# A gated decay recurrence and two MLPs in one kernel: where the decay chain runs, how far it is spread, and how its results are sorted

## What is computed

```python
# attention, per head (B=4, H=8, S=768, D=48), S_re and S_im start at zero
mag = sqrt(a_re**2 + a_im**2);  scale = minimum(mag, 0.999) / (mag + 1e-6)
ar, ai = a_re * scale, a_im * scale
for t in range(S):
    new_re = ar[t] * S_re - ai[t] * S_im
    new_im = ar[t] * S_im + ai[t] * S_re
    S_re, S_im = new_re + outer(k[t], v[t]), new_im
    y[t] = q[t] @ S_re
x = y laid out as (3072 tokens, 384)
# first MLP, d_ff 2048:  h = x @ w_in;  x2 = (h * clip(h + 3, 0, 6) / 6) @ w_out
# second MLP, d_ff 1024: out = ((x2 @ w1) * (x2 @ w2)) @ w3 @ w_out2
```

## Time and profile before

| | us |
|---|---|
| median of 3 runs | 1075.39 (1074.17 to 1079.45) |
| the profiled execution | 1078.01 |
| its span in the profile | 1076.2 |
| until the first g_sb (passes 0 and 1, attention of unit 0) | 133.8 |
| unit 0 | 99.9 |
| units 1 to 5 | 408.7 (86.9, 81.0, 79.9, 81.1, 79.8) |
| unit 6 (attention, no decay chain) | 66.4 |
| unit 7 (neither) | 54.6 |
| second MLP and end | 312.8 |

### The profile page before, as it was taken

One profiled execution on the slowest core, in us unless ns is written; L12 is line 12 of the kernel. 1 busy time (PEld: TensorE's weight loads), 2 busy tenths in 40 slices (PEclk: granted clock), 3 DMA queues, 4 the chain that ended last, 5 costly groups with the idle time before them and its releaser, 6 DMA issues.

```text
span 1076.2 us, 14778 instructions
## 1 busy us (share of the span) xinstructions
...
## 2 busy tenths in 40 slices
...
GB/s 346 137 97 113 168 44 111 68 85 117 66 89 95 84 86 98 84 94 96 78 85 113 70 51 98 37 229 1 52 1 57 2 59 1 59 1 59 1 30 31
DMA packets 85720, 85.85 MB, mean 80 GB/s; under 512 B 8208, under 2 KB 77968, under 8 KB 85648
## 3 DMA queue, kind: packets, MB, share of 16 engines
...
## 4 chain that ended last, share of the span: by engine, by line
issue 35%; PE 31%; POOL 21%; DVE 5%; SPq 2%; ACT 1%; DMA 1%; POOLq 0%; DVEq 0%; ACTq 0%
POOL gL L1309 12%; PE hb L913 9%; PE acc L935 7%; PE bQ L913 5%; PE bR L913 5%; POOL QKs L1297 4%; POOL QKs L1302 3%; PE bP L935 2%; DVE W L1147 1%; POOL woutL L364 1%; PE acc L792 1%; POOL W L1291 1%; POOL W L1289 1%; PE hb L772 1%; DVE W L1139 1%
## 5 line engine op out<-in xcount | busy, mean ns | idle before, releaser
L1309 POOL TENSOR_TENSOR gL<-g_sb,gH 128x384 fp32r<-128x384 f32 x128 | 156.1, 1219 | 355.9 <-ACT gH L1005 355.9
L772 PE MATMUL hb<-xHL,winH 128*128 128x384 f32 x768 | 173.1, 364 | 21.0 <-DMA xHL<-yHL 17.5
L1198 DVE SCALAR_TENSOR_TENSOR g_sb<-t_sb,hb 128x384 f32<-128x384 f32 x128 | 70.4, 550 | 237.5 <-POOL gL L1309 126.4
L772 PEld LDWEIGHTS hb<-xHL,winH 128*128 128x128 f32 x768 | 144.7, 205 | 24.9 <-DMA xHL<-yHL 18.4
L792 PE MATMUL acc<-gH,woutH 128*128 128x384 f32 x384 | 134.5, 350 | 31.8 <-POOL gL L1309 30.9
L1324 POOL TENSOR_TENSOR pL<-p_sb,pH 128x512 fp32r<-128x512 f32 x48 | 67.0, 1396 | 231.9 <-ACT pH L1067 231.9
L792 PE MATMUL acc<-gH,woutL 128*128 128x384 f32 x384 | 134.0, 349 | 0.0
L792 PE MATMUL acc<-gL,woutH 128*128 128x384 f32 x384 | 133.4, 347 | 0.0
L1015 ACT ACTIVATE t_sb<-hb,cst 128x384 f32<-128x384 f32 x128 | 74.4, 581 | 130.3 <-PE hb L772 129.8
L1005 ACT CAST gH<-g_sb 128x384 fp32r<-128x384 f32 x128 | 65.3, 510 | 146.9 <-DVE g_sb L1198 146.8
L792 PEld LDWEIGHTS acc<-gH,woutH 128*128 128x128 f32 x384 | 75.2, 196 | 36.4 <-issue 36.3
...
## 6 DMA issues: line engine op xcount, KB each, us to landing
...
```

Source lines behind the costliest of these rows:

```text
L772: mm = pe.matmul(o, w[:, kk * DF1 + ft * P:kk * DF1 + (ft + 1) * P], xv(u)[:, 2 * kk + part, :], start=(i == 0), stop=(i == 8))
L1198: dve.scalar_tensor_tensor(out=g_sb[:, :], in0=t_sb[:, :], scalar=6.0, in1=hb[n % 2][:, 0:UNIT], op0=ALU.min, op1=ALU.mult).then_inc(s["hs ...
L1309: pool.tensor_tensor(gL[:, (n % 3) * UNIT:(n % 3 + 1) * UNIT], g_sb[:, :], gH[:, (n % 3) * UNIT:(n % 3 + 1) * UNIT].bitcast(F32), ALU.subt ...
```

## The change

Six things, all in the first MLP's part of the program:

1. The products of q and k with the decays and the sine go from POOL to DVE; the squares of passes 2 and later go from POOL to ACT. POOL keeps gL and the low parts of the weights.
2. The angle stays in radians: the offset add (L1139) goes into the scans, which now add two tiles, and a multiplication by 1/pi on ACT comes behind them.
3. The chain is spread: squares at step 0, sums and scans at 4, 6, 7, decays at 8 and 9, products at 10 and 11, wrap at 12, trigonometry at 13, cosine at 14, sine at 15. Unit 0 takes two or three steps in slots 0 to 3 and 15.
4. From unit 0 on YU stands two slots behind S (three for one chunk of unit 0); unit -1 keeps three slots in a row.
5. All 64 blocks of w3 @ w_out2 are multiplied at once; w_out is loaded at slot 0 of unit -1 (before slot 8), and five pieces of the weights are split in unit 0.
6. q and k lie by chunk in QKs and QKc, so that the first two chunks of a pass are sorted by 5 DMAs a half, of double size, the cosine half as soon as it is ready; the third keeps 10. In pass 0 ACT issues the sine half's.

```diff
+        ORDER_W = (0, 4, 1, 5, 2, 6, 3, 7)
+        SPLIT_H = {(-1, 0): (0,), (-1, 8): (4,), (-1, 9): (1,), (0, 1): (5,), (0, 3): (2,), (0, 5): (6,), (0, 7): (3,), (0, 9): (7,)}
...
             if u == 0:
-                return ([(1, sl + 10)] if sl < 4 else []) + ([(2, sl - 2)] if sl >= 3 else [])
+                return {0: [(1, 10), (1, 11)], 1: [(1, 12), (1, 13)], 2: [(1, 14), (1, 15)],
+                        3: [(2, 0), (2, 1)], 15: [(2, 13), (2, 14), (2, 15)]}.get(sl, [(2, sl - 2)])
...
-        W3_MM = {-2: {5: 40}, -1: {0: 3, 1: 3, 2: 3, 3: 3, 4: 2, 5: 2, 6: 2, 7: 2, 8: 4}}
-        W3_COPY = {(-2, 14): (0, 1), (-2, 15): (2, 3, 4), (-1, 3): (5,), (-1, 6): (6,), (-1, 8): (7,)}
+        W3_MM = {-2: {5: FT2 * FT2}}
+        W3_COPY = {(-2, 9): (0, 1), (-2, 10): (2,), (-2, 11): (3, 4), (-1, 0): (5,), (-1, 1): (6,), (-1, 2): (7,)}
...
+        STAGE = {-1: ((0, 3, 6), (1, 4, 7), (2, 5, 8)), 0: ((3, 7, 11), (4, 8, 12), (6, 10, 13))}
...
-            first, step = {-1: (0, 3), 0: (4, 4)}.get(u, (1, 4))
-            j, r = divmod(sl - first - STAGE[stage], step)
+            at_ = STAGE.get(u, ((1, 5, 9), (2, 6, 10), (4, 8, 12)))[("TK", "S", "YU").index(stage)]
...
+            eng.dma_start(f[r:r + D, :, 0:3 * QK], b[0:D, :, :]).then_inc(done, 16)
+            eng.dma_start(f[r:r + D, :, 3 * QK:6 * QK], b[D:D2, :, :]).then_inc(done, 16)
+            eng.dma_start(f[r:r + P - D2, :, 6 * QK:8 * QK], b[D2:P, :, 0:2 * QK]).then_inc(done, 16)
...
-                        if t == 13:
-                            scatter(CPU * p)
-                            scatter(CPU * p + 1)
+                        if t == 14:
+                            scatter_pair(sp, p, 0)
+                        if t == 15 and p > 0:
+                            scatter_pair(sp, p, 1)
...
                 if t == 12:
+                    act.wait_ge(s["turns_summed"], KT * (p + 1))
+                    act.mul(W2[:, :], W1[:, :], float(1 / np.pi)).then_inc(s["turns"], 1)
+                if t == 13:
                     act.wait_ge(s["turns_wrapped"], p + 1)
...
+                if t == 15 and p == 0:
+                    scatter_pair(act, 0, 1)
...
+                    dve.tensor_tensor(part(QKs, 0), part(QKs, 0), tokens(AI), ALU.mult).then_inc(s["q_decayed"], 1)
...
-                    dve.scalar_tensor_tensor(out=W2[:, :], in0=W2[:, :], scalar=float(1 / np.pi), in1=W3[:, :],
-                                             op0=ALU.mult, op1=ALU.add).then_inc(s["turns"], 1)
...
-                        dve.tensor_tensor_scan(W1[:, o], ONE_C.broadcast_to([P, UNIT]), W2[:, o],
-                                               total[:, j:j + 1] if p % 2 else 0.0, ALU.mult, ALU.add).then_inc(s["turns_summed"], 1)
+                        dve.tensor_tensor_scan(W1[:, o], W2[:, o], W3[:, o], total[:, j:j + 1] if p % 2 else 0.0,
+                                               ALU.add, ALU.add).then_inc(s["turns_summed"], 1)
...
+                if t == 15:
+                    dve.wait_ge(s["sin_turns"], p + 1)
+                    for i in range(2):
+                        dve.tensor_tensor(part(QKs, i), part(QKs, i), tokens(W2), ALU.mult).then_inc(s["sin_rotated"], 1)
```

More of the change, by code:

```diff
@@ L59 @@
 FD = 10
+QUARTER_TURN = float(np.float32(np.pi / 4))
 ROUND = 1.5 * 2.0 ** 23
@@ L111, in mixer_mlp_kernel @@
         QKc = at("QKc", KT * CPU * QK)
-        F = [at(f"F{i}", H * QK) for i in range(2)]
+        F2 = at("F2", 2 * H * QK)
+        F = [F2[:, i * H * QK:(i + 1) * H * QK] for i in range(2)]
         Kc = at("Kc", DM + YM - D)
@@ L614, in load_q @@
                 else:
[L615 to L616 removed]
+                    sp.wait_ge(s["f_pair_dma"], 16 * FD * p)
+                    sp.wait_ge(s["f_last_dma"], 16 * FD * p)
                 sp.dma_start(qk(QKs)[:, :, 0:P], qk_src(p, 0)).then_inc(s["q_dma"], 16)
@@ L706, in _ @@
                         store_w3(i)
-                    if u == -1 and sl == 8:
+                    if u == -1 and sl == 0:
                         for i in range(PIECES // 2, PIECES):
@@ L711, in _ @@
                         if g % CPU == 0:
-                            scatter(g + 2)
+                            scatter_last(g // CPU)
                         if g + 2 < NC:
@@ L955, in pre @@
             def pre(p, t):
-                if t == 1 and p <= 1:
+                if t == 0:
                     act.wait_ge(s["a_dma"], 32 * (p + 1))
-                    if p == 1:
-                        act.wait_ge(s["sin_rotated"], 2)
+                    if p > 0:
+                        act.wait_ge(s["sin_rotated"], 2 * p)
                     act.activation(W2[:, :], AI[:, :], ACT.Square).then_inc(s["squares"], 1)
+                    if p > 0:
+                        act.activation(W1[:, :], AR[:, :], ACT.Square).then_inc(s["squares"], 1)
                 if t == 2:
```

189 lines of the change are left out of this document (89 added, 100 removed).

## The result

| | us |
|---|---|
| before, median of 4 runs beside it | 1076.01 (1074.17 to 1079.45) |
| after, median of 4 runs | 1019.91 (1018.55 to 1022.37) |
| ratio | 0.9478, 95% interval 0.9447 to 0.9508 |
| span of after in the profile | 1020.6 |
| until the first g_sb | 105.4 (133.8 before, 105 forecast) |

The kernel is 5.2% faster, 56 us, where 85 were forecast. The time lies in the range by its edge alone, 0.1 under the upper bound where the runs spread over 4, so that it fell inside is luck; and the table says where the other 30 went: the start came out at its number, unit 0 is 15 over it (and longer than before), units 1 to 5 together are 15 over it.

What follows compares the result with a forecast made beforehand. PE was taken as the bound, held up by waits for gL, AT and Ks and a DVE-bound start; 1076.2 - 29 (start) - 10 (unit 0) - 47 (units 1 to 5) = 990; range 965 to 1020.

Steps and rivals of the forecast that it cites:

- The start, -29: Time until the first g_sb: 105 instead of 133.8, by a shorter DVE path, earlier scores and earlier w_out loads.
- ACT's five issues: Pass 0's sine-half sorting: issues take 3.3, landing 2.3, scores at 58.4; help from ACT as second issuing engine worth 3.
- late spot: In unit -1, SP stores w3's last row before the third chunk's sorting; chunk 0's outputs are stored by 79.
- Unit 0, -10: Unit 0 takes 90 against 99.9, including bigger lumps of pass 1 and 2 for splits beside DVE.
- Units 1 to 5, 72.1 each: Each of these units: 66.4 + 3.6 + 1.4 + 0.7; five take 361 against 408.7.
- The base, 66.4: What a unit costs TensorE, read from unit 6, where PE is busy 66.40 of 66.40 us.
- Ks and AT, 1.7 and 4.2, gone: PE's waits in unit 3 for copies Ks (1.7) and masks AT at the outputs (4.2) disappear.
- gL behind the sine products, 3.6, gone: PE's wait for gL behind POOL's sine products, about 2.2 plus 1.4 of clock, goes as DVE takes them.
- gL behind the trigonometry, 3.6, stays: PE's wait for gL behind ACT's trigonometry in slot 13, 2.24 plus 1.4 of clock, remains.
- End of the unit, 1.4 and 0.7: New wait of 1.4 at the unit's first gemm2, behind ACT's squares; possible clock loss of 1.4, counted half.
- Scores of the first chunk: The pair's last sorting DMAs land at 13.4, PE wants them at 14.5: covered by 1.1, otherwise at most 2 late.
- B: Rival: chain stays late through the unit's end, by scans, squares or scores' DMAs; units 77, total 1015; chance 0.16.

Runs made afterwards that it cites:

- eleventh experiment: On the changed kernel, SP also issues pass 0's sine half of the sorting, which ACT issued: 1023.34 us, ratio 0.9497.
- tenth experiment: On the changed kernel, the blocks of w3 @ w_out2, their copies and w_out's loads stand as before the change: 1022.16 us, ratio 0.9494.
- the third: On the changed kernel, ACT issues the sine half's five sorting DMAs in every pass, not in pass 0 alone: 1031.54 us, ratio 0.9571.
- first experiment: On the changed kernel, a pass's first two chunks are sorted one by one, 5 single-size DMAs a half, own semaphores: 994.39 us, ratio 0.9208.
- ninth experiment: All weight pieces split before unit 0, on the kernel with chunks sorted one by one and the sine in slot 14: 977.31 us, ratio 0.9076.
- last experiment: Changed kernel plus single-chunk sorting, later first scores, closer unit 0 stages, sine in slot 14, second square in slot 1, weight splits moved: 960.37 us, ratio 0.8906.
- eighth experiment: On the changed kernel, outputs stand one slot behind the scores again from unit 1 on: 1021.55 us, ratio 0.9454.
- seventh experiment: On the changed kernel, q and k's products with the decays and the sine are POOL's again from pass 2: 1042.92 us, ratio 0.9663.
- first two experiments: Two separate edits of the changed kernel: first two chunks sorted one by one (994.39 us); first chunk's scores one slot later from unit 1 (997.48 us).
- fourth experiment: On the changed kernel, the squares of passes 2 to 7 are POOL's again, behind gL of slot 0: 1022.93 us, ratio 0.9487.

## Why the prediction was right, and where it wasn't

**The start, -29: right, at 105.4.** Its steps held: arctangent done 37.7 (37.2 forecast), scans 40.4 (39.9), cosine products 50.3 (49.9), sine 52.9 (52.6), gemm1 from 101.5 (x landed at 101). One did not: the first scores came at 62.5, not 58.4, because ACT's five issues took 4.9 (3.3 forecast) and the last landed 4.7 behind them (2.3). The late spot that the prediction named did not hide that 4.1: SP's wait for w3's row moves with the scores, as the eleventh experiment shows, and the outputs of chunk 0 were stored by 82.5 instead of 79. The delay was gone when the outputs of chunk 2 ended (95.4 for 95), so the steps of the chain between were forecast some 3 too long; which of them, no run shows. That the start hit its number is two errors that cancel. DVE's products for the sine:

```profile
50.27 2.62 DVE L1202 TENSOR_TENSOR QKs<-QKs,W 128x1152 f32<-128x1152 f32 x2
```

With no POOL work beside them both pairs take 2.6, where the earlier trace rows had 5.85 for the second. The 10 that the prediction gave to w_out's loads, behind the first scores, are borne out in size (10.7 by the tenth experiment, the order of w3's rows included). What it did not set against them is that making all of w3 @ w_out2 at once costs 8.2 ahead of the scores; it had the wait (34) in its steps, but not its price. The rest of the start, 25.9 of 28.4, is the decay chain and the sorting, which no run takes apart.

**ACT's five issues.** I priced the help of the second engine at 3 and wrote that the trace doesn't agree with "small". It is 1.1 by the eleventh experiment, and in the third ACT's issuing in every pass brought nothing. The traces side with the Trainium skill here ("DMA: Bandwidth & Descriptors", Issuing engines are not separate DMA queues): it says that a second engine saves only the time to initiate, usually small beside the DMA. The DMA engines read 0.99 busy while the sine half was under way.

**Unit 0, -10: wrong, +5.** Two steps of it failed. *Sorting*: nothing was put down for it; by the first experiment it is 105.2 - 98.3 = 7. The first scores come behind a wait of 3.9, and gemm1 of two slots on stands behind them in PE's order. *Splits*: "I add 2 for splits beside DVE". By the ninth experiment five pieces in unit 0 are 10.6, their own time on ACT and POOL included, which that run doesn't take apart. The part on DVE shows in the cosine products, with POOL's split beside them:

```profile
124.16 5.84 DVE L1198 TENSOR_TENSOR QKc<-QKs,W 128x1152 f32<-128x1152 f32 x2
```

```profile
123.26 3.46 POOL L398 TENSOR_TENSOR woutL<-woutL_raw,woutH 128x1536 fp32r<-128x1536 f32 x1 [0.38 <-ACT woutH L394]
```

5.84 for 2.62, while the split itself takes 3.46. In the first experiment's kernel PE is past slot 6 of unit 0 at 42 us, where I had 41, and the rest takes 56 instead of 49: there the capping of the logarithm on DVE took 3.18 (0.75 alone) and the scans 6.65 (2.64 alone), both under splits. The prediction had the row that says so, 8.93 for 2.65 in the earlier trace rows, used it for pass 0, where the splits went away, and not for unit 0, where they came.

**Units 1 to 5, 72.1 each: 75.2, by one step.** With chunks sorted one by one they take 72.2. Step by step:

- *The base, 66.4*: right, partly by luck. "PE is busy 66.40 of 66.40 us" was read as what a unit costs TensorE. But unit 6 of before starts at half clock, behind a wait of 3.56 for gL:

```profile
642.00:646.00 4.00, 4.00 (x14) 4.00 (x13) 0.56 (x1) 0.51 (x1) 1.34 (x2) 0.50 0.50 113
```

  and it has 508 matmul records where unit 3 has 529. In the first experiment unit 6 takes 62.2 at full clock. The two errors cancel: in the last experiment, at full clock, unit 3 keeps PE busy for 66.2 (532 records).
- *Ks and AT, 1.7 and 4.2, gone*: right. But of my two reasons for AT one does nothing (eighth experiment).
- *gL behind the sine products, 3.6, gone*: right, one wait for gL is left. Put back on POOL the products cost 3.2 a unit, but by another path, through ACT's squares (seventh experiment).
- *Products at 1.32 to 1.7*: right, 3.43 and 3.44 a pair. Here the row was the better guide than the rule of full exclusion in the Trainium skill ("SBUF — State Buffer", Who interferes with whom), by which I had put a unit at 73 to 74: with sorting out of the way it took 72.2. Under the weight splits it is otherwise, as unit 0 shows.
- *gL behind the trigonometry, 3.6, stays*: right. A wait of 2.10 and then 3.4 us at the level of 1.2 GHz,

```profile
428.65 0.52 PE L816 MATMUL acc<-gH,woutH 128*128 128x384 f32 x1 [2.10 <-POOL gL L1328]
```

```profile
428.80:432.20 3.40, 3.40 (x12) 3.40 (x13) 3.40 (x3) 0.99 (x2) 1.51 (x1) 0.50 0.21 87
```

  and it was 3.2 a unit when it was removed. "Stays" was right of this change and no law: one line moved ends it.
- *End of the unit, 1.4 and 0.7*: the wait for gH is 0.9 to 2.1, as forecast. POOL is busy 19.3 a unit, not 16: gL is stretched by DVE's products, 1.5 for 0.99, without being late by it.
- *Scores of the first chunk*, "the last 5 start at 7.7; 5 x 0.65 and 2.4 to land give 13.4": this is the step that failed. From the first issue of the sine half to the scores it took 445.94 - 436.72 = 9.2, not 5.65: the 0.65 was 0.6 to 1.4, and the 2.4 was 4.7. I had taken issue and landing times from DMAs of half the size, one after the other, and held them for those of a DMA of double size with the cosine half in flight. It is 3.6 late against a cover of 1.1. The wait was bounded at 2 and is 1.2 to 2.7, and I had put no clock loss behind it: 3.4 us at half clock are 1.7 more. Since the wait for gH grows when the one for F goes, the two net to 3 a unit.

The rival that came nearest is B, chain late through the end of the unit, at 1015: it named "the scores' DMAs" among three causes, and the first two experiments single it out. The scans were as forecast (3.42 and 3.54). The squares cost nothing that shows while F is late (fourth experiment); with F there, a square moved to slot 1 goes with slots 0 and 1 falling from 7.3 to 6.4 (last experiment). The total lies 0.1 inside the range, with unit 0 and units 1 to 5 both 15 over; the start, right by errors that cancel, kept it there.

**Not settled.** What the long DMAs cost by size and what by number in flight was not separated. Of the splits' 10.6 in unit 0, it is open how much is DVE's and how much stands ahead of gH and gL. And no run has w_out's early loads without ACT's wait for w3's first row; by the tenth experiment that wait is worth up to 8.2 at the first scores.
